# Another order of the stages of an attention pair, and the w_out loads issued by ScalarE

## The chip, the cores and the metric

The kernel runs on 1 core of one Trainium2 chip. The time is the device time of one execution in microseconds (us): 1208.38 us is the median of 3 runs of the kernel before (1195.93 to 1210.83). Everything that is said of its inside comes from one profiled execution of it.

## The reference

Three layers follow one another, all in float32.

- Attention over q, k, v of (4 batches, 8 heads, 768 tokens, 64): for each chunk of 32 queries, scores against 8 memory keys and a window of 56 keys, softmax, product with the values. Its output is laid out as 3072 tokens of 512.
- A gated layer: `sigmoid(x @ w_gate) * (x @ w_val) @ w_out`, with 512 to 1536 and back to 512.
- A rational layer: `h = x @ w_in` (512 to 2048), `g = P(h) / (Q(h) + 1e-6)` with P cubic and Q from |h| and h*h, then `g @ w_out`.

The output is (3072, 512) float32.

## The kernel before, in words

The engines run programs written out by hand, which meet at semaphores. Products that need full precision are made as three passes: each operand is split into a rounded part ("hi", a copy made by ScalarE) and the rest ("lo", a subtraction made by VectorE), and TensorE adds hi\*hi, hi\*lo and lo\*hi.

**Phases.** The tokens are worked off in NS = 3 stages of two blocks of 512 tokens. At the start, `attention(0)` runs alone on TensorE, with small products on the identity matrix between its parts (`warm_up`, L1117). Then comes for each stage s a run of six quads (`quad_a`, on TensorE two `chain` calls each), which make the gated layer's first products by a scheme with seven products (`STEPS`), and between the quads the thirds of the w_out products. Between two stages stands a **middle**: `attention(8 * (s + 1))` for the next tokens, with 30 of 36 remaining thirds of this stage between its parts, and the rest behind it. There are two middles. After the third stage the w_out products of the last blocks run while the weights of the rational layer are loaded and split (`split_b`), and then the rational layer runs to the end (`block_b`).

**An attention pair.** `attention` on TensorE (L1204) works off 8 units (a batch and half the heads' layout for 128 tokens each) in four pairs p = 0 to 3, with units a and b. For a unit there are: `scores` (64 small matmuls, L1086), on VectorE `softmax` without the exponent (a reduce L732, a subtract L735), on ScalarE `exp_scores` (L402), then the first `turn` (4 transposes, L1099), `copy_turned` on ScalarE (L408), `weigh_values` (64 small matmuls, L1111), on VectorE `normalize` (L743 to L747), the second `turn` (`turn(g, False)`), and `stage_x` on ScalarE (L418). `fill` is either one warm-up of three products or one third: four matmuls with 512 columns. Both units have buffers of their own; `scores` of unit g waits for `stage_x` of unit g - 2 (L1075).

**w_out pieces.** w_out is streamed as 72 pieces of 256 KB (12 per block), into a ring of ORING = 3 raw slots (`oraw`) and a ring of 3 split slots (`wout`). `load_oraw(n)` (L257) is issued by SyncE and waits until VectorE has made the lo part of piece n - 3 (`wo_lo`), since that reads the raw slot. `split_wout(n)` on ScalarE (L442) makes the hi part, on VectorE (L788) the lo part. A piece has three thirds on TensorE, and the first waits for its lo part (L1180). In the middles the pieces are split at the places that `at_middle(p, place)` names; on ScalarE place 0 lies between `copy_turned(a)` and `exp_scores(b)`, place 1 between that and `copy_turned(b)`, place 2 at the end of the pair. On VectorE place 0 lies between `softmax(a)` and `softmax(b)`, place 1 behind `normalize(a)`. `last_operands` splits what the next quads need, with three places `between(0)` to `between(2)` in which pieces n + 11 to n + 13 are split; n is the piece with which the middle begins.

SyncE's queue carries all transfers in program order: q, k and v of the units, the gated layer's weights (`load_raw`), the w_out pieces, the stores of finished blocks and the rational layer's weights.

Of the kernel before, what the change touches and what calls it, by code (L numbers as in the profile page):

```python
# [26 lines left out]
TA, TB = FA // P, FB // P  # L27
# [28 lines left out]
ORING = 3  # L56
# [12 lines left out]
def build(nc, q, k, v, wgv, wo, wb, coef_a, coef_b, y_dram, out):  # L69
    with ExitStack() as ctx:  # L70
# [168 lines left out]
        def _(sp):  # L239
# [58 lines left out]
            load_oraw(0)  # L298
            load_oraw(1)

            for s in range(NS):
                for i in range(NQ):
                    c, n = CHAINS * s + 2 * i, first_piece(s, i)
                    load_raw(c + 2)
                    load_oraw(n + 4)
# [7 lines left out]
                    load_oraw(n + 5)  # L313
# [6 lines left out]
                load_oraw(n + 4)  # L320
                load_qk(g + 2)
                load_oraw(n + 5)
                load_qk(g + 3)
                load_v(g + 2)
                store_a(2 * s, 0)
                store_a(2 * s, 1)
                load_oraw(n + 6)
                store_a(2 * s, 2)
                store_a(2 * s, 3)
                load_v(g + 3)  # L330
                for p in (1, 2):
                    load_qk(g + 2 * p + 2)
                    load_oraw(n + 2 * p + 5)
                    load_oraw(n + 2 * p + 6)
                    load_qk(g + 2 * p + 3)
                    load_v(g + 2 * p + 2)
                    load_v(g + 2 * p + 3)
                for ahead in range(11, 16):
                    load_oraw(n + ahead)
# [3 lines left out]
            load_oraw(n + 4)  # L343
            load_braw(B_EARLY + 1)
            load_oraw(n + 5)
# [4 lines left out]
            load_oraw(n + 6)  # L350
            for m in range(4):
                store_a(NT - 2, m)
            for ahead in range(7, TA + 2):
                load_braw(B_EARLY + ahead - 4)
                load_oraw(n + ahead)
# [42 lines left out]
        def _(act):  # L398
# [181 lines left out]

            attention(0, at_start)
            nc.scalar.preload_act_table_set("sigmoid_and_others")
# [7 lines left out]
            for s in range(NS - 1):  # L590
# [4 lines left out]
                def at_middle(p, place):  # L595
                    if place == 0:
                        split_wout(n + 2 * p + 2)
                        if p:
                            split_wout(n + 2 * p + 3)
                    if p == 0:  # L600
                        if place == 1:
                            copy_out_a(2 * s, 0)
                            copy_out_a(2 * s, 1)
                        elif place == 2:
                            split_wout(n + 3)
                            split_w(c, 0)
                    elif p == 1:
                        if place == 1:
                            split_w(c, 1)
                        elif place == 2:  # L610
                            split_w(c, 2)
                            split_w(c, 3)
                    elif p == 2:
                        if place == 2:
                            split_x(s + 1, B11)
                    elif place == 0:
                        split_x(s + 1, B21)
                    elif place == 2:
                        split_wout(n + 10)
                        split_x(s + 1, T2, 0)  # L620
# [4 lines left out]
                nc.scalar.preload_act_table_set("sigmoid_and_others")  # L625
# [101 lines left out]
        def _(dve):  # L727
# [168 lines left out]
            def last_operands(s, between):  # L896
                split_x(s, T2, 0)
# [3 lines left out]
                between(0)  # L901
# [470 lines left out]
```

## Time and profile before

| what | value |
|---|---|
| median of 3 runs | 1208.38 us (1195.93 to 1210.83) |
| the profiled execution, its own time | 1207.63 us |
| its span | 1205.3 us |
| TensorE busy | 1172.7 us (97%) |
| VectorE busy | 905.0 us (75%) |
| ScalarE busy | 751.3 us (62%) |
| GpSimd busy | 121.4 us (10%) |
| moved by DMA | 97.79 MB |

The span runs from the first to the last instruction; the time of the execution is 2.3 us longer. TensorE's busy time counts matmuls that overlap, so its idle time is read from single rows and not from the share. Its clock is shown as a share of full speed: 1.00 is 2.4 GHz and 0.50 is 1.2 GHz.

### The profile page before, as it was taken

Reading aid. Unit: us, or ns where it says so; the run is one execution under the profiler, and the core shown is the slowest. Engines: PE = TensorE matmul, PEld = TensorE weight load, DVE = VectorE, ACT = ScalarE, POOL = GpSimd, SP = SyncE. Lnnn points to the kernel's source line nnn. Section 1 sums busy time; section 2 is a strip of 40 time slices with the busy share of each in tenths; the row PEclk is TensorE's granted clock in tenths of the full one; section 3 lists DMA queues with packets and bytes.
Section 4 is the critical chain, followed back from the end, with each engine's and each line's share of the span. In section 5 each row is a group of like instructions: output and inputs, shape, how many; then the busy total and the mean of one; then the engine's idle time right before and its main releaser. Section 6 shows DMA issues by size and latency. Waiting matters only on the chain.

```text
span 1205.3 us, 21070 instructions
## 1 busy us (share of the span) xinstructions
PE 1172.7 (97%) x8160; PEld 962.8 (80%) x8160; DVE 905.0 (75%) x1387; ACT 751.3 (62%) x1224; POOL 121.4 (10%) x150
## 2 busy tenths in 40 slices
PE   8899999989999987999999999999999999999998
PEld 7778887768888765788887888888888888888887
DVE  3675666667566644676657899998998998988987
ACT  2464555455555533555555787777877877877875
POOL 2122222003322200223200000000000000000000
PEclk9999999999999998999999999999999999999999
DMA  8412422833242172332207400200200100100000
GB/s 285 150 53 79 141 70 71 277 100 110 79 140 79 63 246 100 99 133 84 90 24 248 171 1 1 70 1 1 70 0 0 70 0 0 70 0 0 36 1 35
DMA packets 40720, 97.79 MB, mean 81 GB/s; under 512 B 4288, under 2 KB 4288, under 8 KB 40640
## 3 DMA queue, kind: packets, MB, share of 16 engines
q1 hardware_dynamic: 40640, 96.68, 23.6%
q8 instruction: 55, 0.90, 0.3%
q14 instruction: 25, 0.20, 0.1%
HBM read 84.09 MB, written 12.58 MB: 80 GB/s over the span
## 4 chain that ended last, share of the span: by engine, by line
PE 91%; DVE 3%; ACT 2%; issue 2%; DMA 1%; SPq 0%; ACTq 0%; DVEq 0%
PE ps_h L1151 9%; PE ps_h L1158 9%; PE ps_h L1153 9%; PE ps_h L1257 7%; PE ps_h L1262 7%; PE ps_h L1258 7%; PE ps_y L1301 7%; PE ps_y L1295 7%; PE ps_y L1297 7%; PE ps_y L1196 4%; PE ps_y L1201 4%; PE ps_y L1197 4%; PE ps_h L1099 2%; PE ps_h L1086 1%; PE ps_h L1111 1%
## 5 line engine op out<-in xcount | busy, mean ns | idle before, releaser
L1151 PE MATMUL ps_h<-xop,wop 128*128 128x512 f32 x504 | 197.0, 391 | 1.8 <-DVE x_raw L806 1.5
L1153 PE MATMUL ps_h<-xop,wop 128*128 128x512 f32 x504 | 196.1, 389 | 0.0
L1158 PE MATMUL ps_h<-xop,wop 128*128 128x512 f32 x504 | 155.9, 390 | 0.0
L1257 PE MATMUL ps_h<-x_split,weights 128*128 128x512 f32 x384 | 149.4, 389 | 0.0
L1258 PE MATMUL ps_h<-x_split,weights 128*128 128x512 f32 x384 | 149.4, 389 | 0.0
L1295 PE MATMUL ps_y<-weights,hid 128*128 128x512 f32 x360 | 140.0, 389 | 0.0
L1297 PE MATMUL ps_y<-weights,hid 128*128 128x512 f32 x360 | 140.0, 389 | 0.0
L785 DVE TENSOR_TENSOR wop<-rawp,wop 128x448 fp32r<-128x448 f32 x144 | 91.3, 665 | 47.7 <-ACT wop L439 47.7
L1196 PE MATMUL ps_y<-hid,wout 128*128 128x512 f32 x264 | 109.9, 416 | 7.6 <-DVE wout L790 7.4
L806 DVE TENSOR_TENSOR x_raw<-ps_h,probs_t 128x512 f32<-128x512 f32 x72 | 49.5, 688 | 87.3 <-PE ps_h L1158 87.1
L672 ACT ACTIVATE tmp<-ps_h 128x512 f32<-128x512 f32 x96 | 57.1, 595 | 92.5 <-PE ps_h L1262 92.5
L1151 PEld LDWEIGHTS ps_h<-xop,wop 128*128 128x128 f32 x504 | 94.6, 188 | 23.4 <-DVE x_raw L806 2.4
L1153 PEld LDWEIGHTS ps_h<-xop,wop 128*128 128x128 f32 x504 | 94.7, 188 | 20.1
L1158 PEld LDWEIGHTS ps_h<-xop,wop 128*128 128x128 f32 x504 | 94.6, 188 | 19.7
L1197 PE MATMUL ps_y<-hid,wout 128*128 128x512 f32 x264 | 105.8, 401 | 0.0
L1262 PE MATMUL ps_h<-x_split,weights 128*128 128x512 f32 x384 | 102.6, 389 | 0.0
L1301 PE MATMUL ps_y<-weights,hid 128*128 128x512 f32 x360 | 96.2, 389 | 0.0
L1006 DVE TENSOR_TENSOR tmp<-tmp 128x512 f32<-128x512 f32 x96 | 66.1, 688 | 30.4 <-ACT tmp L675 30.4
L481 ACT ACTIVATE hid<-x_raw 128x512 fp32r<-128x512 f32 x72 | 45.4, 630 | 64.8 <-DVE x_raw L820 64.8
L790 DVE TENSOR_TENSOR wout<-oraw,wout 128x512 fp32r<-128x512 f32 x72 | 52.0, 730 | 44.2 <-ACT wout L446 44.2
L1257 PEld LDWEIGHTS ps_h<-x_split,weights 128*128 128x128 f32 x384 | 72.1, 188 | 15.0
L1262 PEld LDWEIGHTS ps_h<-x_split,weights 128*128 128x128 f32 x384 | 72.1, 188 | 15.0
(90 smaller groups left out, 2285.8 us busy)
## 6 DMA issues: line engine op xcount, KB each, us to landing
rawp<-wgv_l SPq DMA_DIRECT2D x36, 512.0 KB, 3.5
oraw<-wo_l SPq DMA_DIRECT2D x72, 256.0 KB, 3.6
unit<-v_l SPq DMA_DIRECT2D x24, 520.0 KB, 6.0
unit<-k_l SPq DMA_DIRECT2D x24, 512.0 KB, 5.6
unit<-q_l SPq DMA_DIRECT2D x24, 256.0 KB, 4.1
x_stage<-y_dram SPq DMA_DIRECT2D x6, 1024.0 KB, 5.8
out<-stage SPq DMA_DIRECT2D x24, 256.0 KB, 2.2
braw<-wb_l SPq DMA_DIRECT2D x11, 512.0 KB, 6.2
```

What stands on the lines that cost most here:

```text
L785: nc.vector.tensor_tensor(wop[:, c % 2, 1, cols], rawp[:, c % 2, 256 + 448 * i:256 + 448 * (i + 1)], wop[:, c % 2, 0, cols].bitcast(F32), ...
L1151: nc.tensor.matmul(dst, w_h[k], xop[:, m, 0, k, :], start=first and k == 0, stop=False, skip_group_check=True)
L1153: nc.tensor.matmul(dst, w_l[k], xop[:, m, 0, k, :], start=False, stop=False, skip_group_check=True)
L1158: last = nc.tensor.matmul(dst, w_h[k], xop[:, m, 1, k, :], start=False, stop=k == 1, skip_group_check=True)
L1196: nc.tensor.matmul(ps_y[:, m, :], w_at(0, m), h[0], start=f == 0, stop=False)
L1197: nc.tensor.matmul(ps_y[:, m, :], w_at(1, m), h[0], start=False, stop=False)
L1257: nc.tensor.matmul(dst, lhs(c, 0), x_split[:, 0, c, :], start=(c == 0), stop=False)
L1258: nc.tensor.matmul(dst, lhs(c, 1), x_split[:, 0, c, :], start=False, stop=False)
L1262: last = nc.tensor.matmul(dst, lhs(c, 0), x_split[:, 1, c, :], start=False, stop=(c == KT - 1))
L1295: nc.tensor.matmul(ps_y[:, m, :], hid_b(i, 0)[:, P * m:P * (m + 1)], wb_at(i, 1, 0), start=(i == 0), stop=False)
L1297: nc.tensor.matmul(ps_y[:, m, :], hid_b(i, 0)[:, P * m:P * (m + 1)], wb_at(i, 1, 1), start=False, stop=False)
L1301: nc.tensor.matmul(ps_y[:, m, :], hid_b(i, 1)[:, P * m:P * (m + 1)], wb_at(i, 1, 0), start=False, stop=False)
```

## The change

The order of a pair on TensorE: `scores(b)` follows directly on `turn(a, True)`; two fills stand between `scores(b)` and `weigh_values(a)`; `turn(a, False)` stands behind `weigh_values(b)`. The number of fills per pair stays. `load_oraw` moves from SyncE to ScalarE: pieces 0 and 1 are loaded first of all, and each `split_wout(n)` on ScalarE begins with `load_oraw(n + 2)`, wait included. The places of the splits in the middles change on ScalarE and VectorE, `between(0)` comes first in `last_operands`, and the load of the sigmoid table comes behind it.

```diff
@@ sync @@
-            def load_oraw(n):
-                if n >= PIECES:
-                    return
-                wait(sp, wo_lo, n - ORING + 1)
-                sp.dma_start(oraw[:, n % ORING, :], wo[n % TA]).then_inc(oraw_loaded[n % ORING], 16)
...  (all calls of load_oraw on SyncE are gone, the other issues keep their order)
@@ scalar @@
+            def load_oraw(n):
+                if n >= PIECES:
+                    return
+                wait(act, wo_lo, n - ORING + 1)
+                act.dma_start(oraw[:, n % ORING, :], wo[n % TA]).then_inc(oraw_loaded[n % ORING], 16)
+
             def split_wout(n):
+                load_oraw(n + 2)
                 act.wait_ge(oraw_loaded[n % ORING], 16 * (n // ORING + 1))
...
             def last_operands(s, between):
+                between(0)
+                nc.scalar.preload_act_table_set("sigmoid_and_others")
                 split_x(s, T3, 0)
                 split_x(s, T4, 0)
-                between(0)
...
+            load_oraw(0)
+            load_oraw(1)
             attention(0, at_start)
-            nc.scalar.preload_act_table_set("sigmoid_and_others")
...
                 def at_middle(p, place):
-                    if place == 0:
+                    if p < 2 and place == 0:
                         split_wout(n + 2 * p + 2)
-                        if p:
-                            split_wout(n + 2 * p + 3)
...
+                        split_wout(n + 2 * p + 3)
+                    elif p == 0 and place == 1:
+                        copy_out_a(2 * s, 0)
+                        copy_out_a(2 * s, 1)
+                    elif p == 0:
+                        split_w(c, 0)
+                    elif p == 1 and place == 1:
+                        split_w(c, 1)
                     elif p == 1:
+                        split_w(c, 2)
+                        split_w(c, 3)
+                        split_wout(n + 6)
+                    elif p == 2 and place == 0:
+                        split_wout(n + 7)
+                    elif p == 2 and place == 1:
+                        split_x(s + 1, B11)
                     elif p == 2:
+                        split_wout(n + 8)
+                        split_wout(n + 9)
                     elif place == 0:
                         split_x(s + 1, B21)
+                    elif place == 1:
                         split_wout(n + 10)
@@ vector @@
             def last_operands(s, between):
+                between(0)
                 split_x(s, T2, 0)
                 split_x(s, T1, 0)
                 token_sum(s, T3, 0)
                 token_sum(s, T4, 0)
-                between(0)
...
                 def at_middle(p, place):
                     if place == 0:
                         split_wout(n + 2 * p + 2)
-                        if p:
-                            split_wout(n + 2 * p + 3)
+                        split_wout(n + 2 * p + 3)
+                        if p == 3:
+                            token_sum(s + 1, T1, 0)
...
@@ tensor @@
                     turn(a, True)
-                    fill()
                     scores(b)
-                    weigh_values(a)
                     fill()
                     fill()
+                    weigh_values(a)
                     turn(b, True)
-                    turn(a, False)
+                    fill()
                     fill()
                     weigh_values(b)
+                    turn(a, False)
                     fill()
```

## Rows read from the trace of the kernel before

**Rows 1.** Windows: us, busy us (instructions) of each engine, TensorE clock, DMA share, GB/s.
```profile
0.00:60.00 60.00, 50.51 (x1301) 46.06 (x1302) 30.56 (x56) 23.39 (x39) 10.88 (x18) 0.97 0.66 218
211.00:291.00 80.00, 76.24 (x1255) 60.27 (x1254) 52.63 (x91) 41.11 (x74) 7.40 (x8) 0.98 0.49 167
421.00:515.00 94.00, 81.11 (x1254) 63.28 (x1253) 52.86 (x93) 41.31 (x73) 6.99 (x8) 0.93 0.44 147
642.00:680.00 38.00, 37.60 (x164) 30.16 (x163) 30.55 (x35) 26.68 (x37) 0.00 (x0) 1.00 0.78 279
```
**Rows 2.** Waits, whole span: who waited for whom, us in total, times, longest.
```profile
PE ps_y L1196 <- DVE wout L790: 7.4, 5, 1.9
PE ps_h L1111 <- issue: 7.4, 4, 3.5
PE ps_h L1086 <- issue: 7.0, 3, 3.6
```
**Rows 3.** TensorE's timeline, first middle: start, us, and the idle time before.
```profile
234.37 0.60 PE L1099 MATMUL ps_h<-ident,probs 128*128 128x128 f32 x4
237.27 0.50 PE L1196 MATMUL ps_y<-hid,wout 128*128 128x512 f32 x1
239.50 1.09 PE L1099 MATMUL ps_h<-ident,probs 128*128 128x128 f32 x8
243.38 1.14 PE L1086 MATMUL ps_h<-unit 64*32 64x64 f32 x64
249.39 0.50 PE L1196 MATMUL ps_y<-hid,wout 128*128 128x512 f32 x1 [1.93 <-DVE wout L790]
264.85 0.50 PE L1196 MATMUL ps_y<-hid,wout 128*128 128x512 f32 x1 [1.64 <-DVE wout L790]
```
**Rows 4.** ScalarE's timeline in the same pair.
```profile
235.01 0.60 ACT L408 ACTIVATE probs_t<-ps_h 128x512 f32<-128x512 f32 x1 [0.36 <-PE ps_h L1099]
235.50 1.14 ACT L446 ACTIVATE wout<-oraw 128x512 fp32r<-128x512 f32 x2
238.81 0.63 ACT L402 ACTIVATE probs<-probs 128x512 f32<-128x512 f32 x1 [2.17 <-DVE probs L735]
```
**Rows 5.** VectorE's timeline in the same pair, and a lo pair before it.
```profile
223.99 1.29 DVE L790 TENSOR_TENSOR wout<-oraw,wout 128x512 fp32r<-128x512 f32 x2 [2.66 <-ACT wout L446]
236.16 1.29 DVE L790 TENSOR_TENSOR wout<-oraw,wout 128x512 fp32r<-128x512 f32 x2 [2.66 <-ACT wout L446]
237.37 0.68 DVE L732 TENSOR_REDUCE row_stats<-ps_h 128x8 f32<-128x512 f32 x1
238.09 0.69 DVE L735 TENSOR_TENSOR probs<-ps_h,row_stats 128x512 f32<-128x512 f32 x1
```
**Rows 6.** SyncE's queue, first middle: issues and how long each held the queue.
```profile
212.84 0.33 SPq L261 DMA_DIRECT2D oraw<-wo_l  x1
213.69 1.77 SPq L244 DMA_DIRECT2D unit<-k_l  x1
224.71 0.93 SPq L261 DMA_DIRECT2D oraw<-wo_l  x2
```
**Rows 7.** TensorE's timeline, start and second middle: stalls named issue, the first wait.
```profile
5.78 0.85 PE L1086 MATMUL ps_h<-unit 64*32 64x64 f32 x64 [1.32 <-DMA unit<-k_l]
38.61 0.30 PE L1111 MATMUL ps_h<-unit,probs_t 64*32 64x65 f32 x2 [3.53 <-issue]
433.95 0.63 PE L1086 MATMUL ps_h<-unit 64*32 64x64 f32 x37 [3.60 <-issue]
475.63 0.43 PE L1111 MATMUL ps_h<-unit,probs_t 64*32 64x65 f32 x25 [2.31 <-issue]
```
**Rows 8.** Windows of 2 us, columns as in the first group.
```profile
251.00:253.00 2.00, 2.00 (x97) 1.73 (x94) 1.62 (x4) 0.00 (x0) 0.00 (x0) 0.50 0.61 224
265.00:267.00 2.00, 2.00 (x9) 1.65 (x10) 1.21 (x3) 0.78 (x2) 0.00 (x0) 1.00 0.53 126
432.00:434.00 2.00, 0.05 (x7) 0.05 (x11) 0.00 (x0) 0.00 (x0) 0.00 (x0) 1.00 1.03 391
436.00:438.00 2.00, 2.00 (x9) 1.71 (x8) 0.04 (x1) 1.23 (x2) 0.00 (x0) 0.50 0.95 344
```
**Rows 9.** TensorE's timeline, start: the two first turns of the second pair.
```profile
21.50 0.66 PE L1099 MATMUL ps_h<-ident,probs 128*128 128x128 f32 x4 [0.20 <-ACT probs L402]
25.96 1.09 PE L1099 MATMUL ps_h<-ident,probs 128*128 128x128 f32 x8 [0.15 <-ACT probs L402]
```

More of the change, by code:

```diff
@@ L319, in _ @@
                 n, g = piece_of(s, 0, TA - 2), UNITS * (s + 1)
-                load_oraw(n + 4)
                 load_qk(g + 2)
-                load_oraw(n + 5)
                 load_qk(g + 3)
                 load_v(g + 2)
[L325 to L329, printed above, removed]
-                load_v(g + 3)
[L331 to L339, printed above, removed]
+                for m in range(4):
+                    store_a(2 * s, m)
+                load_v(g + 3)
+                load_qk(g + 4)
+                load_qk(g + 5)
+                load_v(g + 4)
+                load_v(g + 5)
+                load_qk(g + 6)
+                load_qk(g + 7)
+                load_v(g + 6)
+                load_v(g + 7)
             n = piece_of(NS - 1, 0, TA - 2)
             load_braw(B_EARLY)
-            load_oraw(n + 4)
             load_braw(B_EARLY + 1)
-            load_oraw(n + 5)
             for m in range(4):
@@ L349, in _ @@
             load_braw(B_EARLY + 2)
-            load_oraw(n + 6)
             for m in range(4):
                 store_a(NT - 2, m)
-            for ahead in range(7, TA + 2):
-                load_braw(B_EARLY + ahead - 4)
-                load_oraw(n + ahead)
+            for o in range(B_EARLY + 3, TB - 1):
+                load_braw(o)
             load_braw(TB - 1)
@@ L595, in at_middle @@
                 def at_middle(p, place):
-                    if place == 0:
+                    if p < 2 and place == 0:
                         split_wout(n + 2 * p + 2)
-                        if p:
-                            split_wout(n + 2 * p + 3)
[L600 to L606, printed above, removed]
-                    elif p == 1:
[L608 to L612, printed above, removed]
+                        split_wout(n + 2 * p + 3)
[6 more added lines that the diff above has]
+                        split_w(c, 1)
+                    elif p == 1:
+                        split_w(c, 2)
[5 more added lines that the diff above has]
+                        split_x(s + 1, B11)
                     elif p == 2:
-                        if place == 2:
-                            split_x(s + 1, B11)
+                        split_wout(n + 8)
+                        split_wout(n + 9)
                     elif place == 0:
                         split_x(s + 1, B21)
-                    elif place == 2:
+                    elif place == 1:
                         split_wout(n + 10)
+                    else:
                         split_x(s + 1, T2, 0)
@@ L958, in at_middle @@
                     else:
+                        token_sum(s + 1, T2, 0)
                         split_x(s + 1, B21)
                         split_wout(n + 10)
-                    if p == 3 and place == 0:
-                        token_sum(s + 1, T1, 0)
-                        token_sum(s + 1, T2, 0)
                 attention(UNITS * (s + 1), at_middle)
```

8 lines of the change are left out of this document (1 added, 7 removed).

## The prediction

> **What bounds the kernel now.** I read the windows by stage first, then the table of waits, then TensorE's timeline of the start and the middles beside those of ScalarE, VectorE and SyncE's queue. TensorE is the bound nearly everywhere: from 642 to 680 us it idles 0.4 us [rows 1], and in the rational layer behind 680 us, which the change does not touch, it runs back to back. What the change can reach is the start (60 us, 9.5 us idle), the first middle (80 us, 3.8 idle) and the second (94 us, 12.9 idle, at a mean clock of 0.93) [rows 1]. The two middles hold the same instructions, so the 14 us between them are stalls. Three kinds of idle time make up most of it [rows 2]: 7.4 us in which a third waits for the lo part of its w_out piece, and 14.4 us of "issue", in which TensorE stands still inside its runs of 64 small matmuls with nothing to wait for: 7.4 us in `weigh_values` (4 times) and 7.0 us in `scores` (3 times). An idle stretch costs twice: after the 1.93 us one [rows 3] the clock stands at 0.50, that is 1.2 GHz, and after the 3.60 us one [rows 7] too [rows 8]. Each such stretch at 1.2 GHz lasted about 4 us, so about 2 us are lost each time. After the 1.64 us idle time [rows 3] the clock stayed at 1.00 [rows 8]. I take the price of an idle stretch over 1.9 us as itself plus up to 2 us.
>
> The sum is made against the profiled execution, 1207.63 us, which is 0.75 us below the median.
>
> **The pair on TensorE.** Stage lengths from the first middle, start to start: a turn 0.36 us, scores or weigh before a fill 0.78, a fill about 1.03, or 1.1 before small matmuls. Between the first turn of a and the first turn of b TensorE now has a fill, scores, weigh and two fills, and the pair takes 5.13 us there (234.37 to 239.50 [rows 3]), the last half microsecond of it waiting. Changed, it has 0.36 + 0.78 + 1.03 + 1.10 + 0.78 = 4.05 us of work there: one fill less. The chain that runs beside it on the other engines is what decides. From the same rows: turn a to `copy_turned` 0.64, copy to the first hi 0.49 [rows 4], that to the first lo 0.66, two lo parts to the reduce 1.21, reduce to subtract 0.72, subtract to exp 0.72, exp to the turn of b 0.69 [rows 3 to 5]. That is the 5.13 us.
>
> **The new wait.** In p = 0 and p = 1 ScalarE splits two pieces at place 0, and the second `split_wout(m + 1)` now begins with `load_oraw(m + 3)`, which waits for the lo part of piece m. So hi, lo, hi, lo run one behind the other instead of overlapping. Queued behind that wait on ScalarE are the second hi and exp(b); VectorE waits for the hi with softmax(b) behind it, and TensorE's turn of b waits for exp(b). SyncE's issue came 0.72 us after the start of the lo part (223.99 to 224.71 [rows 5, 6]) and held its queue 0.33 us [rows 6]; the trace has no issue on ScalarE, so I take that. The chain becomes 0.64 + 0.49 + 0.66 + (0.72 + 0.37) + 0.66 + 0.60 + 0.72 + 0.72 + 0.69 = 6.27 us, and TensorE idles 2.2 us. From the turn of b to the next pair it then has 0.36 + 1.0 + 1.1 + 0.78 + 0.36 + 1.1 = 4.7 us. So p = 1 takes 10.97 us from the turn of a, against 8.99 now (about +2.0), and p = 0, where one piece is split now, +2.2. In p = 2 one hi is left in the chain: 4.52 us against 4.05, +0.2 for the pair.
>
> **What the other places give back.** In p = 3 the pieces' hi parts are made in p = 2 already, so the 1.93 us wait and its half clock go: the stretch from turn a to the last turn was 13.0 us and becomes 9.65, -3.35. With `between(0)` first, piece n + 11 is ready and the 1.64 us wait goes: -1.8 with what lay around it. Per middle 2.2 + 2.0 + 0.2 - 3.35 - 1.8 = -0.75, for both -1.5. The four new idle stretches of 2.2 us may each be followed by half clock: 0 to 8 us, since 1.64 us left the clock alone and 1.93 did not. I take half, +3.8.
>
> **The start.** Warm-ups cover the waits there. The first turn of a to that of b is 4.46 us (21.50 to 25.96 [rows 9]) and has one split in it; TensorE's new work is about 3.55, so 0.9 us of waiting, 0.15 of it there already, in two pairs, and 0.5 in the last: +2.0. The two w_out loads that ScalarE issues at once add 0.5 MB to the first burst, before the q and k loads for which TensorE already waits 1.32 us [rows 7]. At the 391 GB/s of a full stretch [rows 8] that is 1.3 us at most, 0 at least; I take +1.2, since both loads are in flight when the first scores need k.
>
> **Moves at no price.** In the quads ScalarE gets 0.33 us per issue, six microseconds apart, beside the idle time in which it waits for TensorE; without that cover it would be up to 50 x 0.33 = 16 us. The loads are issued two pieces ahead, about 8 us in the middles against a landing of some 3.6 us; behind 642 us TensorE needs 5.4 us for two pieces, and 0.3 us of wait may go or come. SyncE loses 72 issues, and none of its q, k, v loads waits behind a `wo_lo` wait any longer; v of a comes one and a half microseconds later by the later weigh, but is needed a pair later. The table load moves behind one more split and keeps two steps of the first chain as cover. Scores of the next a now stand only a fill behind `turn(a, False)`: 0.36 + 1.1 us against 0.64 + 0.6 + 0.1 for `stage_x`, no wait, by 0.1 us.
>
> **The issue stalls.** The long ones end as a burst of transfers drains (391 GB/s from 432 to 434 us [rows 8]), and the instructions between two neighbouring ones come to about 256, so I read them as the fetch of the next block of instructions. Four of the seven lie in `weigh_values` directly behind `scores`, where 256 instructions go by in 1.44 us. Changed, no two of these runs touch, and 256 instructions take 2.9 us at least. I count these four as gone: 0.96 + 3.53 + 0.55 + 2.31 = 7.35 us and 4 us of half clock behind two of them, -11.3. Bounds: nothing gone, 0; all seven gone, 7.0 us and some 5.5 us of half clock more, -24.
>
> The Trainium skill ("Runtime: NRT & Kernel Launch", Instruction fetch mechanics) says that TensorE's instruction memory is refilled in 16 KiB blocks of 256 instructions, that it holds 2048, and that crossing a block is mostly hidden. By that the spacing of two runs would not matter, and the -11.3 would be 0; the trace agrees on the 256 and not on the hiding, with stalls of 3.5 us.
>
> **Sum.** 1207.63 - 1.5 + 3.8 + 2.0 + 1.2 - 11.3 = 1201.8, so 1202 us.
>
> **Rivals.** (1) The stalls go by the bursts alone, and stay: the first middle had a busy DMA and none, which speaks for chance; that `weigh_values` behind `scores` has four of seven speaks weakly against. 1202 + 11.3 = 1213 us. (2) All seven go, since the new idle stretches give the fetch time: 1202 - 12.5 = 1189 us. (3) The new wait on ScalarE does not bite, because the second issue runs ahead of what I assume: 1202 - 4 x 2.2 - 3.8 = 1189 us; with rival 2 on top 1177, over 2% faster. The wait is in the program and its lo part in the trace, which speaks against. (4) Slower than before: ScalarE's issues are held up as SyncE's was for 1.77 us [rows 6], in the four serial chains at place 0, and each is followed by half clock while the stalls stay. 1213 + 4 x 1.44 + 3.8 = 1223 us; it decides against the forecast once an issue takes over 1.3 us (or over 0.33 with the stalls kept). For over 2% slower both middles must also stall as the second does now (+14): 1237. The Trainium skill ("DMA: Bandwidth & Descriptors", Arbitration) says that each DMA engine takes turns between the queues that have work for it; that would bring the w_out loads past the k and v bursts, and by it this rival would lose its ground, but an own landing time of a ScalarE load is in no row here.
>
> **Chances.** Forecast 0.40 (1195 to 1208 by itself), rival 1 0.27, rival 2 0.13, rival 3 0.10, rival 4 0.10. The range 1187 to 1217 holds the first four but for the meeting of 2 and 3, and leaves out rival 4. A difference of 2%, 24 us, is about what a measurement of this kernel can tell from no change: faster by over 2% 0.05, slower 0.04, within 0.91.
>
> **What would show it.** Right: the turn of b follows the turn of a by about 6.3 us in p = 0 and 1 of both middles, with some 2.2 us of idle time put down to exp; no wait for wout in p = 3 and behind the attention; ScalarE's own queue with issues of 0.33 us; no issue stall in `weigh_values`. Wrong: issue stalls as long as before at other places; no idle time at the turn of b; a first `scores` at the same 5.78 us; waits in the quads for `snapshot` copies, which would mean that ScalarE's issues are not covered.

## The result and the profile after

The changed kernel is slower: 1209.22 us median of 20 runs (1205.3 to 1213.09), against 1201.44 us of 20 runs of the kernel before (1195.93 to 1210.95). The ratio is 1.0054, interval 1.0036 to 1.0073. The forecast was 1202 us and a range up to 1217: the time lies in the range, the direction was wrong.

The two profiled executions show the opposite, 1207.63 us before and 1205.3 after. That is the first thing to see: the profiled execution of before stood 6 us above the median that more runs gave, and the sum was made against it. That of the changed kernel stood 4 us below its median and is the fastest of its 20 runs, so what the two profiles show side by side flatters the change by 10 us. The page of the changed kernel:

```profile
span 1202.9 us, 21070 instructions
PE 1169.1 (97%) x8160; PEld 957.6 (80%) x8160; DVE 901.8 (75%) x1387; ACT 752.5 (63%) x1224; POOL 118.7 (10%) x150
q10 hardware_dynamic: 10368, 18.88, 5.1%
oraw<-wo_l ACTq DMA_DIRECT2D x72, 256.0 KB, 2.7
```

The w_out loads have a queue of their own (q10) and land after 2.7 us instead of 3.6. The windows of the start and the two middles, columns as in [rows 1]:

```profile
0.00:60.00 60.00, 48.74 (x1278) 42.96 (x1279) 27.16 (x52) 21.65 (x36) 9.18 (x18) 1.00 0.65 214
211.00:291.00 80.00, 72.79 (x1242) 56.21 (x1241) 49.24 (x86) 38.92 (x68) 6.45 (x8) 1.00 0.53 172
421.00:515.00 94.00, 83.78 (x1342) 64.63 (x1341) 58.96 (x102) 44.15 (x77) 8.08 (x8) 0.98 0.49 159
```

The waits over the whole span, which answer to [rows 2]:

```profile
PE ps_h L1087 <- ACT probs L382: 15.8, 17, 2.1
PE ps_y L1184 <- DVE wout L780: 2.3, 1, 2.3
PE ps_h L1087 <- DVE probs L737: 2.3, 3, 1.5
```

The issue stalls sum to 3.6 us where they were 14.4, the waits for wout to 2.3 where they were 7.4; in their place stand 15.8 us of waiting for exp (1.8 before). From TensorE's timelines, first scores to first chain: the first middle went from 61.8 to 63.4 us, the second from 76.0 to 66.0 (it had the long stalls), the start to the first chain from 60.3 to 62.9, the six quads between the middles from 148.3 to 149.3, and all behind the second middle from 713.2 to 715.8. The six quads ahead of the first middle took 145.6 us in both. So each stretch that the change reaches got longer except the one in which that execution of before had stalled most.

### The profile page after: what moved, and what is told of

Same layout as the page of the kernel before. It is cut to its first block, busy times and chain, and to the rows that moved or that the text cites. A ratio compares the mean times of both kernels' runs of the same rounds, so it can differ in the third digit from the quotient of the medians.

```text
span 1202.9 us, 21070 instructions
## 1 busy us (share of the span) xinstructions
PE 1169.1 (97%) x8160; PEld 957.6 (80%) x8160; DVE 901.8 (75%) x1387; ACT 752.5 (63%) x1224; POOL 118.7 (10%) x150
## 4 chain that ended last, share of the span: by engine, by line
PE 90%; DVE 5%; ACT 3%; issue 2%; DMA 0%; ACTq 0%; SPq 0%; DVEq 0%
PE ps_h L1139 9%; PE ps_h L1146 9%; PE ps_h L1141 9%; PE ps_h L1245 7%; PE ps_h L1250 7%; PE ps_h L1246 7%; PE ps_y L1283 7%; PE ps_y L1289 7%; PE ps_y L1285 7%; PE ps_y L1184 4%; PE ps_y L1185 4%; PE ps_y L1189 4%; PE ps_h L1087 2%; PE ps_h L1099 1%; PE ps_y L1107 1%
## 5 line engine op out<-in xcount | busy, mean ns | idle before, releaser
L775 DVE TENSOR_TENSOR wop<-rawp,wop 128x448 fp32r<-128x448 f32 x144 | 88.4, 644 | 58.2 <-ACT wop L419 58.2
L1184 PE MATMUL ps_y<-hid,wout 128*128 128x512 f32 x264 | 107.3, 406 | 2.5 <-DVE wout L780 2.3
L1185 PE MATMUL ps_y<-hid,wout 128*128 128x512 f32 x264 | 104.3, 395 | 0.0
L1246 PEld LDWEIGHTS ps_h<-x_split,weights 128*128 128x128 f32 x384 | 72.1, 188 | 15.0
L1250 PEld LDWEIGHTS ps_h<-x_split,weights 128*128 128x128 f32 x384 | 72.1, 188 | 15.0
L1245 PEld LDWEIGHTS ps_h<-x_split,weights 128*128 128x128 f32 x384 | 72.0, 188 | 14.9
```

What stands on the lines that cost most here:

```text
L775: nc.vector.tensor_tensor(wop[:, c % 2, 1, cols], rawp[:, c % 2, 256 + 448 * i:256 + 448 * (i + 1)], wop[:, c % 2, 0, cols].bitcast(F32), ...
L1184: nc.tensor.matmul(ps_y[:, m, :], w_at(0, m), h[0], start=f == 0, stop=False)
L1185: nc.tensor.matmul(ps_y[:, m, :], w_at(1, m), h[0], start=False, stop=False)
L1245: nc.tensor.matmul(dst, lhs(c, 0), x_split[:, 0, c, :], start=(c == 0), stop=False)
L1246: nc.tensor.matmul(dst, lhs(c, 1), x_split[:, 0, c, :], start=False, stop=False)
L1250: last = nc.tensor.matmul(dst, lhs(c, 0), x_split[:, 1, c, :], start=False, stop=(c == KT - 1))
```

## The new waits, each in its rows

**Hi, lo, hi, lo in series.** TensorE in the first middle: the first turn of a and that of b in pair 1, the first turn of a in pair 3, the last turn, and the first chain.

```profile
227.19 0.60 PE L1087 MATMUL ps_h<-ident,probs 128*128 128x128 f32 x4
233.53 0.66 PE L1087 MATMUL ps_h<-ident,probs 128*128 128x128 f32 x4 [2.12 <-ACT probs L382]
256.13 0.65 PE L1087 MATMUL ps_h<-ident,probs 128*128 128x128 f32 x4 [1.24 <-ACT probs L382]
265.90 0.60 PE L1087 MATMUL ps_h<-ident,probs 128*128 128x128 f32 x4
271.84 0.39 PE L1139 MATMUL ps_h<-xop,wop 128*128 128x512 f32 x1
```

The turns stand 6.34 us apart (6.40 in pair 0) against 5.13 in [rows 3], with 2.12 us of idle time. ScalarE and its queue (ACTq) in the same pair:

```profile
227.82 0.60 ACT L388 ACTIVATE probs_t<-ps_h 128x512 f32<-128x512 f32 x1 [0.35 <-PE ps_h L1087]
227.83 0.33 ACTq L426 DMA_DIRECT2D oraw<-wo_l  x1
228.32 0.62 ACT L433 ACTIVATE wout<-oraw 128x512 fp32r<-128x512 f32 x1
229.70 0.33 ACTq L426 DMA_DIRECT2D oraw<-wo_l  x1
230.13 0.63 ACT L433 ACTIVATE wout<-oraw 128x512 fp32r<-128x512 f32 x1 [1.19 <-DVE wout L780]
232.85 0.63 ACT L382 ACTIVATE probs<-probs 128x512 f32<-128x512 f32 x1 [2.08 <-DVE probs L725]
```

VectorE in the same pair, the first lo part:

```profile
228.97 0.69 DVE L780 TENSOR_TENSOR wout<-oraw,wout 128x512 fp32r<-128x512 f32 x1 [2.65 <-ACT wout L433]
```

The first issue runs beside the copy and costs nothing. The second comes at 229.70 us, only when VectorE has made the lo part (228.97 to 229.66), and the second hi stands behind it; in [rows 4] both hi parts ran back to back.

**Exp of pair 3.** ScalarE at the end of pair 2 (first middle), where `split_wout(n + 9)` was put:

```profile
254.50 0.33 ACTq L426 DMA_DIRECT2D oraw<-wo_l  x1
254.93 0.63 ACT L433 ACTIVATE wout<-oraw 128x512 fp32r<-128x512 f32 x1 [3.09 <-PE ps_y L1189]
255.47 0.61 ACT L382 ACTIVATE probs<-probs 128x512 f32<-128x512 f32 x1
```

The issue of piece n + 11 waits for the lo part of n + 8, which VectorE makes behind softmax(a) of pair 3 (253.78 to 254.46 us), and exp(a) stands behind it: the 1.24 us wait at 256.13 above. The row names TensorE as releaser, but the issue that holds the hi part back came less than 0.1 us behind VectorE's lo part.

**The start.** First rows of ScalarE, then of VectorE, between the second and the third pair, then of TensorE: the first scores, the two turns at the third pair, and the last turn of all:

```profile
32.15 0.60 ACT L398 ACTIVATE x_raw<-ps_h 128x512 f32<-128x512 f32 x1 [2.12 <-PE ps_h L1087]
32.65 0.57 ACT L419 ACTIVATE wop<-rawp 128x448 fp32r<-128x448 f32 x1
```
```profile
33.25 0.63 DVE L775 TENSOR_TENSOR wop<-rawp,wop 128x448 fp32r<-128x448 f32 x1 [4.02 <-ACT wop L419]
34.83 0.68 DVE L722 TENSOR_REDUCE row_stats<-ps_h 128x8 f32<-128x512 f32 x1
```
```profile
6.60 1.17 PE L1074 MATMUL ps_h<-unit 64*32 64x64 f32 x64 [2.13 <-DMA unit<-k_l]
34.97 0.66 PE L1087 MATMUL ps_h<-ident,probs 128*128 128x128 f32 x4 [0.41 <-DVE probs L737]
36.95 0.66 PE L1087 MATMUL ps_h<-ident,probs 128*128 128x128 f32 x4 [0.66 <-ACT probs L382]
59.83 0.66 PE L1087 MATMUL ps_h<-ident,probs 128*128 128x128 f32 x4 [1.51 <-DVE probs L737]
```

`turn(a, False)` now stands behind `weigh_values(b)`, so `stage_x(a)` on ScalarE comes late, and behind it in program order the hi part of the gated layer's weights. VectorE has the matching lo part in front of `normalize(b)` and of the next `softmax`. So the later turn costs at the next pair's two turns (0.41 and 0.66 us), on engines where nothing had moved. In the kernel before the same chain had ended in time: ScalarE's `stage_x(a)`, VectorE's lo part, and TensorE's turn of the last b with no wait, then that of a:

```profile
27.14 0.59 ACT L418 ACTIVATE x_raw<-ps_h 128x512 f32<-128x512 f32 x1
28.23 0.62 DVE L785 TENSOR_TENSOR wop<-rawp,wop 128x448 fp32r<-128x448 f32 x1 [1.95 <-ACT wop L439]
30.86 0.60 PE L1099 MATMUL ps_h<-ident,probs 128*128 128x128 f32 x4
32.34 0.66 PE L1099 MATMUL ps_h<-ident,probs 128*128 128x128 f32 x4 [0.20 <-ACT probs L402]
```

The last turn waits 1.51 us for `normalize` (0.60 before). The first scores come at 6.60 us instead of 5.78 [rows 7].

**Behind the second middle.** TensorE in the first chain of the last quads:

```profile
492.32 0.50 PE L1184 MATMUL ps_y<-hid,wout 128*128 128x512 f32 x1 [2.29 <-DVE wout L780]
493.90 0.50 PE L1139 MATMUL ps_h<-xop,wop 128*128 128x512 f32 x1 [0.37 <-ACT probs_t L440]
```

The wait for piece n + 11 behind the attention (1.64 us in [rows 3]) is gone, and TensorE reaches piece n + 12 earlier, which waits for the same row of splits and sums on VectorE and ScalarE. Behind the second middle the gain is given back, and 1 us more. Behind the first no wait for wout came; a wait of 0.39 us stands in its first quad, and the six quads take 1.0 us more, so part of the gain stays there.

## The experiments

Each ratio is against runs of the kernel before on the same chip. Differences between experiments go by ratios; 0.001 is 1.2 us. The changed kernel has 20 runs, e7 and e9 have 8, e11 and e12 have 6, the others 12. The last column is the distance from the lowest run to the median; it depends on the number of runs, and for the kernel before it was 5.5, 6.3, 7.5 and 4.7 us in the other comparisons. The standard deviation is steadier: 4.2 to 5.0 us for the kernel before in each comparison, 2.0 for the changed one.

| kernel | median us | ratio and interval | lowest to median |
|---|---|---|---|
| before (35 runs of one comparison) | 1203.48 | | 9.8 |
| changed | 1209.22 | 1.0054 (1.0036 to 1.0073) | 3.9 |
| e1 order only | 1207.77 | 1.0028 (1.0006 to 1.0051) | 2.1 |
| e2 loads only | 1202.98 | 0.9985 (0.9960 to 1.0009) | 4.8 |
| e3 first loads late | 1207.46 | 1.0042 (1.0016 to 1.0067) | 2.6 |
| e4 load behind hi | 1200.98 | 0.9981 (0.9950 to 1.0012) | 3.0 |
| c1 before again | 1203.78 | 1.0000 (0.9969 to 1.0031) | 5.8 |
| e5 old order at the start | 1203.14 | 0.9987 (0.9960 to 1.0014) | 3.5 |
| e6 loads on SyncE | 1197.62 | 0.9983 (0.9961 to 1.0004) | 1.1 |
| e7 before, earlier splits | 1196.79 | 0.9924 (0.9893 to 0.9955) | 7.1 |
| e8 e7, loads on ScalarE | 1195.32 | 0.9947 (0.9923 to 0.9971) | 3.9 |
| e9 small loads | 1192.60 | 0.9941 (0.9918 to 0.9964) | 0.7 |
| e10 runs apart, same cover | 1201.27 | 0.9979 (0.9953 to 1.0005) | 6.6 |
| e11 e7 and e10 | 1190.49 | 0.9913 (0.9885 to 0.9942) | 2.0 |
| e12 changed, e3 + e4 + e5 | 1195.90 | 0.9891 (0.9848 to 0.9933) | 4.7 |
| e13 changed, piece n + 9 later | 1208.37 | 1.0015 (0.9987 to 1.0043) | 3.5 |

**e1, the order alone.** Only TensorE's pair order of the changed kernel, in the kernel before.

> The kernel before with TensorE's new pair order alone (loads on SyncE, splits where they were). Theory A (the new order has one fill too few between the two first turns, 4.05 us of work for a chain of 5.13 us, and the issue stalls are small in a typical run): about 1.1 us of wait for exp at the turn of b in p = 1 to 3 of both middles, +0.6 us a pair net, some +3.5 us in the start; +6 us against before in all. Rival B (the order pays, because the issue stalls shrink, and the cost of the change lies in ScalarE's loads): no slower than before, -3 to 0 us, and fewer issue stalls in the profile.

Slower by 3.4 us of the forecast 6. The sign speaks against rival B: the order does not pay by itself. Its profile has 9.4 us of waiting for exp in all and 8.8 us of issue stalls, fewer than the 14.4 of before, as rival B had said.

**e2, the loads alone.** `load_oraw` on ScalarE in front of each split, in the kernel before.

> The kernel before with the w_out loads issued by ScalarE alone (old pair order, splits where they were). Theory A (the load in front of the second of two neighbouring splits waits for the first one's lo part, so hi, lo, hi, lo run in series): the turn of b comes 6.3 us after the turn of a in p = 1 to 3 instead of 5.13, +1.2 us each, +7 us, and +2 us at the start from the two first loads; +9 us. Theory C (the issues themselves on ScalarE cost, 0.33 us x 72, wherever they stand): waits of TensorE spread over the quads as well, and more than +9. Rival B: +9 too. Rival D (the order alone is what costs): 0 to +2 us.

Measured -1.8 us, no difference, where theory A said +9. The mechanism is there: the turns stand 6.34 us apart in pairs 1 and 2, and the first middle takes 64.65 us instead of 61.81. But the old order had 5.1 us of cover, so only 1.33 us of each 6.34 is idle. In its profile the waits for exp rose by 5.6 us (7.4 against 1.8; some 7 were forecast), and the issue stalls were 8.9 us against 14.4. So the serial wait is there, and something of nearly its size came back. That the own queue is what brings the stalls down is not shown: e8 has the same queue and 12.4 us of them.

**e3, the first two loads late.**

```diff
-            load_oraw(0)
-            load_oraw(1)
             attention(0, at_start)
+            load_oraw(0)
+            load_oraw(1)
```

> The changed kernel, with the loads of pieces 0 and 1 issued behind the first attention instead of ahead of it. Theory A (0.5 MB of w_out share the DMA engines with the first q and k): first scores back at 5.8 us instead of 6.6, no half clock behind it, -2 us against the changed kernel. Rival: the first scores are as late without them, by the landing of k alone, 0 us.

The first scores came at 5.25 us instead of 6.60. They came at 6.16 to 6.60 us in the five profiles in which ScalarE loads pieces 0 and 1 first of all, and at 5.01 to 5.78 in the eleven others, so the mechanism is shown; the time went from 1.0054 to 1.0042, 1.4 us, inside the intervals.

**e4, the load behind the hi part.**

```diff
             def split_wout(n):
-                load_oraw(n + 2)
                 act.wait_ge(oraw_loaded[n % ORING], 16 * (n // ORING + 1))
...
                 nc.scalar.activation(wout[:, n % ORING, 0, :], oraw[:, n % ORING, :], ACT.Copy).then_inc(wo_hi, 1)
+                load_oraw(n + 2)
```

> The changed kernel, with load_oraw(n + 2) behind the hi part of split_wout(n) instead of in front of it: the same issues and the same semaphore, but no hi part stands behind the wait. Theory A (serial chain): the turn of b follows the turn of a by 5.1 to 5.3 us in p = 0 and 1 instead of 6.34 to 6.40, so 4 x 1.1 = -4.5 us against the changed kernel; the 1.24 us wait in p = 3 stays, since exp(a) still stands behind the load of n + 11. Theory C (issue time as such): 0 us, the waits stay at 2.1 us.

From 1.0054 to 0.9981: one moved line gives 8.8 us. TensorE's two turns of pair 1 in the first middle:

```profile
230.31 0.60 PE L1087 MATMUL ps_h<-ident,probs 128*128 128x128 f32 x4
235.43 0.66 PE L1087 MATMUL ps_h<-ident,probs 128*128 128x128 f32 x4 [0.93 <-ACT probs L382]
```

5.12 us, as forecast, with the same 72 issues on ScalarE: issuing there costs nothing, the wait in front of the hi part does. The four chains give 4.9 us, and the wait in pair 3, which was expected to stay at 1.24, fell to 0.71 and 0.65 us, 1.1 us more. Some 3 us are left over. A part of it is the clock. In the changed kernel the first such wait of the second middle (2.11 us, ending at 431.94 us) is followed by half clock, the one of the first middle is not:

```profile
430.00:432.00 2.00, 0.06 (x1) 0.06 (x2) 1.90 (x5) 0.74 (x2) 0.00 (x0) 1.00 1.01 359
434.00:436.00 2.00, 2.00 (x47) 1.25 (x51) 0.50 (x1) 0.00 (x0) 0.00 (x0) 0.50 0.97 371
```

So an idle stretch of 2.1 us sometimes costs itself alone and sometimes 1.7 us more. The changed kernel, e3, e5 and e13 have four such waits each in pairs 0 and 1 of their middles: 7 of these 16 were followed by half clock, 1, 2, 2 and 2. In e4's middles no wait for exp is above 0.93 us and none is followed by half clock; its 2.27 us wait for piece n + 12, behind the second middle, is.

**c1, the kernel before again.**

> The kernel before against itself: a ratio of 1.00 within its interval, and a second profile of it. Theory S (its issue stalls are a lottery of each run: its runs spread from 1193.7 to 1216.3 us, and the profiled one stood high in them): the second profile has issue stalls at other places or of another sum than 14.4 us, and the first middle and the other stages agree with the first profile to 0.3 us where no stall falls. Rival: the stalls sit at fixed places in every run, and the same seven come back.

The ratio is 1.0000. Its issue stalls, from TensorE's timeline:

```profile
37.24 0.30 PE L1111 MATMUL ps_h<-unit,probs_t 64*32 64x65 f32 x2 [2.72 <-issue]
245.38 0.34 PE L1086 MATMUL ps_h<-unit 64*32 64x64 f32 x13 [2.28 <-issue]
256.58 0.54 PE L1111 MATMUL ps_h<-unit,probs_t 64*32 64x65 f32 x35 [1.19 <-issue]
427.66 0.34 PE L1111 MATMUL ps_h<-unit,probs_t 64*32 64x65 f32 x12 [0.56 <-issue]
436.92 0.87 PE L1086 MATMUL ps_h<-unit 64*32 64x64 f32 x37 [2.79 <-issue]
466.49 0.30 PE L1086 MATMUL ps_h<-unit 64*32 64x64 f32 x4 [3.17 <-issue]
477.71 0.66 PE L1111 MATMUL ps_h<-unit,probs_t 64*32 64x65 f32 x25 [1.62 <-issue]
```

Half right and half wrong for both sides. Where a stall comes is fixed: a run stops with 2, 37 and 25 of its 64 matmuls to go, just as in [rows 7]. Whether it comes, and how long it lasts, is not: the first middle has two here and had none, two of the start are missing. The sum is 14.3 us again, and this profiled execution (1210.18 us) too stood 6 us above the median of its kernel.

Two more readings tell what these stalls are. Counted in matmuls from the first, the stalls of the start come behind number 222, 349, 858 or 985, in all 16 profiles and in every order of the pair. They are 127 or 509 matmuls apart; 127 matmuls with their weight loads are 254 instructions, and a few waits stand between them. And each page of the profile lists a queue for instructions (packets, MB, share of the DMA engines), here that of before, and the same queue from 431.5 to 432.0 us, inside the 3.60 us stall of [rows 7]:

```profile
q8 instruction: 55, 0.90, 0.3%
q8 instruction: 1, 0.02, 11.9%
```

These are 55 packets of 16 KB. The one in that stall ran from 431.61 to 432.57 us, and TensorE went on at 433.95. All 94 stalls named issue in the 16 profiles end 1.1 to 1.7 us after such a packet has landed. So the stalls are waits for the next block of instructions, which the prediction had only read from the counts. The packets behind these stalls took 0.9 to 1.5 us, one took 2.3. A long stall is one whose packet started late: that of the 3.60 us stall started 1.26 us after TensorE had stopped. Why it starts late is open.

**e5, the old order at the start.** `attention` takes the old order for `first == 0`.

> The changed kernel with the old pair order in the first attention alone. Theory A (the new order has one warm-up too few over each chain, and the waits for exp and for normalize add up to 6.2 us in the profile of the changed kernel against 1.4 before): the start shortens by 4 to 5 us, and so does the time. Rival (the start is set by the landing of q, k and v, whatever the order): 0 to -1 us.

From 1.0054 to 0.9987, 8 us (6 by medians), more than theory A's 4 to 5, and the first chain starts at 56.76 us instead of 62.92. Of these 6.2 us, 0.2 lie ahead of the first scores and 0.5 in issue stalls. The forecast had +2.0 us for the order there.

**e6, the loads back on SyncE**, with order and places as changed.

> The changed kernel with the w_out loads back on SyncE at the places where the kernel before issues them; TensorE's order and the places of the splits as changed. Theory A: both serial waits on ScalarE go, turn a to turn b 5.1 to 5.3 us in p = 0 and 1, no 1.24 us wait in p = 3, and the first scores come at 5.0 to 5.8 us; -7 us and more against the changed kernel, 1201 to 1203 us. Rival (the order's missing fill is nearly the whole cost): at most -3 us, 1206 and above.

0.9983 and 1197.62 us: -8.5 us. More than what the changed kernel loses against before (6.5 us) goes with the load in ScalarE's queue in front of the hi part, and e4 gets the same back without moving the loads away. The rival is out. But e5 gets as much back at the start, so this is not the only cause: the changed kernel carries both costs, and its gains elsewhere cover one of them.

**e7, the kernel before with earlier splits.** Only what the change does well: piece n + 8 at the end of pair 2, `between(0)` first.

```diff
                     if place == 0:
-                        split_wout(n + 2 * p + 2)
+                        if p < 3:
+                            split_wout(n + 2 * p + 2)
...
                     elif p == 2:
-                        if place == 2:
+                        if place == 1:
                             split_x(s + 1, B11)
+                        elif place == 2:
+                            split_wout(n + 8)
```

> The kernel before (order and loads untouched) with the two late pieces split earlier: piece n + 8 at the end of pair 2, between(0) first in last_operands with the table load behind it. Theory A: the 1.93 us wait and the 2 us of half clock behind it go in both middles, and that is kept, -7 us; the 1.64 us wait goes from its place, but comes back in the first chain of the next quads as a wait for piece n + 12, 0 us. Rival (what was forecast): the 1.64 us are kept as well, -11 us.

-9.1 us by the ratio, -7.0 by medians, between the two theories and settling neither. The first middle takes 58.8 us instead of 61.8, and the quads behind it 0.4 us more; all behind the second middle takes 2.4 us more (715.6 against 713.2). That speaks for theory A, though not by a wait at piece n + 12: the waits for wout are 0.9 us in all.

**e8, e7 with the loads behind the hi part on ScalarE.**

> The kernel before with the earlier splits of e7, and the w_out loads issued by ScalarE behind each hi part, the first two behind the first attention. Theory A (the issue itself is covered, and only hi parts queued behind the load's wait cost; the own queue thins out the bursts, so fewer issue stalls): 1193 to 1196 us, narrower spread than e7. Theory C (issues on ScalarE cost as such): above 1199 us.

1195.3 us as theory A said, but by the ratio no better than e7 (0.9947 and 0.9924, intervals overlapping), and with 12.4 us of issue stalls in its profile against 10.5 in that of e7. That the own queue gives fewer stalls is not borne out.

**e9, small loads.** From the third unit on only 64 columns of q, k and v are loaded.

> The kernel before, which from the third unit on loads only 64 columns of q, k and v (so it computes with old data; the program and all semaphores are the same). Theory F2 (issue stalls are instruction fetches held up by bursts of data on the same DMA engines): no stall above 0.3 us in the profile, the half clock behind them gone, the runs within 2 to 3 us of each other at 1193 us or a little below, -9 us against before. Rival (the fetch itself is too slow for 256 instructions in 1.44 us, whatever else moves): the stalls come back at their places, and the spread stays.

It runs at 1192.6 us within 4 us from lowest to highest. Its stalls in the second middle, and, with columns as in [rows 1], the microsecond in which TensorE stops for the last:

```profile
419.20 0.34 PE L1113 MATMUL ps_h<-unit,probs_t 64*32 64x65 f32 x12 [0.69 <-issue]
426.54 0.63 PE L1088 MATMUL ps_h<-unit 64*32 64x64 f32 x37 [0.87 <-issue]
451.95 0.30 PE L1088 MATMUL ps_h<-unit 64*32 64x64 f32 x4 [0.46 <-issue]
462.12 0.44 PE L1113 MATMUL ps_h<-unit,probs_t 64*32 64x65 f32 x25 [2.57 <-issue]
459.00:460.00 1.00, 0.55 (x50) 0.38 (x38) 0.82 (x2) 0.00 (x0) 0.00 (x0) 1.00 0.88 330
```

The same four places. Two are far shorter (3.60 to 0.87 us, 2.62 to 0.46), two are not (0.55 and 0.69, 2.31 and 2.57). In front of the longest one the DMA engines are busy all the same (share 0.88, 330 GB/s): two w_out loads, which were not made smaller, run there, and the block of instructions starts at 459.63 us. So the bursts of q, k and v lengthen the stalls and make them vary; they do not make them. Without them the kernel is 7 us faster, of which the profile shows 8.5 us less of stalls than in before (5.9 against 14.4). Both theories were too simple.

**e10, the runs apart with the same cover.**

```diff
                     turn(a, True)
                     fill()
                     scores(b)
-                    weigh_values(a)
-                    fill()
                     fill()
+                    weigh_values(a)
+                    fill()
                     turn(b, True)
-                    turn(a, False)
                     fill()
+                    turn(a, False)
                     weigh_values(b)
```

> The kernel before with one edit on TensorE: in a pair the three fills between the two first turns are dealt out as fill, scores(b), fill, weigh(a), fill, so that the two runs of 64 small matmuls do not touch but the work between the turns stays 4.6 us and more. Theory F (issue stalls are instruction fetches that cannot keep up with 256 instructions in 1.44 us beside a burst of transfers): the spread of its runs narrows to that of the changed order (2 to 5 us from the lowest to the median instead of 10) with the lowest at 1194 to 1196, so a median of some 1198, -5 us. Rival G (the stalls go by the bursts alone): same median and spread as before. Rival H (they shrank in the changed kernel only because TensorE idled more and gave the fetch its time): same as before too, but the order alone, with its waits, had less.

-2.5 us with an interval that holds zero: inconclusive. The stalls in its profile are 10.0 us, 1.7 of them in `weigh_values` (7.4 in before) and 8.3 in `scores` (7.0), and the places in the start are again behind matmuls 349, 858 and 985. That the neighbourhood of the two runs makes the stalls, on which -11.3 us of the forecast rested, is not shown: where they come goes by the count.

**e11, e7 and e10 together.**

> The kernel before with the earlier splits of e7 and the fills dealt out as in e10. If the two gains add: 1196.8 - 2.5 = 1194 us. If what e10 gave was chance: 1197 us. If normalize or the lo parts are pushed into each other by both: above 1198 us, with a wait for wout in p = 3.

1190.49 us, 0.9913 (0.9885 to 0.9942): faster than both kernels, 1.4% below the changed one. Against e7 the intervals overlap, so whether e10's part adds is open. Its profile, taken in the slowest of its six runs, has 7.1 us of issue stalls, that of e7 10.5.

**e12, three mends together**: e3, e4 and e5 in the changed kernel.

> The changed kernel with three of its parts undone or mended together: the load behind the hi part (as in e4), the old pair order in the first attention (as in e5), the first two loads behind that attention (as in e3). Theory A (three separate waits that add up: -8.2, -6.1 and -1.8 us by medians against the changed kernel): some 1193 to 1196 us, below the kernel before. Rival (they overlap, one hides the other, for instance since any idle time lets the instruction fetch catch up and its loss brings issue stalls back): 1199 to 1202 us, and more issue stalls in its profile than the changed kernel's 3.6 us.

0.9891 (0.9848 to 0.9933). Against the changed kernel this is -0.0163; the three single steps give -0.0012, -0.0073 and -0.0067, together -0.0152. Within the intervals they add. The changed kernel without these three is faster than the one before. Its profile has 7.1 us of issue stalls against 3.6 in the changed one, as the rival had it; one profile each does not tell whether that is more than chance.

**e13, piece n + 9 later.**

> The changed kernel with one split moved in the middles on ScalarE: piece n + 9 from the end of pair 2 to place 0 of pair 3, so that exp(a) of pair 3 no longer stands behind the load of piece n + 11, which waits for the lo part of n + 8. Theory A: the 1.24 us wait at the first turn of a in p = 3 goes in both middles, and nothing takes its place, -2.5 us against the changed kernel. Rival (the chain is only moved: hi of n + 9 and the B21 split now stand before exp(b)): the wait comes back at the turn of b in p = 3, 0 us.

The wait at the first turn of a goes, and this stands at that of b in pair 3, first middle (1.67 us in the second):

```profile
266.19 0.66 PE L1087 MATMUL ps_h<-ident,probs 128*128 128x128 f32 x4 [1.45 <-ACT probs L382]
```

By the rows the rival is right, the wait is moved. The ratio (1.0015) lies lower than the changed kernel's, with intervals that just overlap; I go by the rows.

## Why the prediction was wrong, point by point

The steps that failed: the credit for stalls was counted on an execution 6 us above the typical one, the order in the start was priced at a third of its cost, and three waits were put at nothing, those in front of the first turn of a in pairs 2 and 3 and that at piece n + 12.

- **The profiled execution as the base: wrong.** The sum started at 1207.63 us. More runs put the median at 1201.44, and the three runs shown (1195.93 to 1210.83) had said that single executions differ by 15 us. Both profiles of this kernel, with 14.4 and 14.3 us of stalls, come from executions 6 us above their medians. A credit for stalls taken from one high execution is only worth what the typical one has of them.
- **The new wait in pairs 0 and 1: right in size.** 6.27 us forecast, 6.40 and 6.34 measured, 2.2 us of idle time forecast and 2.1 measured, the issue of 0.33 us right. Half clock behind half of these was right too: 7 of 16 in four profiles.
- **Pair 2 from the turn of a on: right** (9.31 us to the next scores, 9.01 before; +0.2 forecast).
- **What the other places give back: the step that failed in the middles.** Turn a to the last turn takes 9.77 us (9.65 forecast), and from turn a of pair 3 to the chain it is 5.16 us less than before in the first middle, 5.15 forecast. But the text priced each pair from turn a on and did not ask what stood in front of it. From scores(a) to the first turn of a pair 2 takes 3.98 us (3.18 before) with a wait of 0.41, and pair 3 takes 4.58 (3.48 before) with the 1.24 us behind the load of n + 11: 1.9 us in the first middle, and the same two waits stand in the second. So the first middle became 1.5 us longer, where the sum had -0.75 ahead of its +3.8 for half clock, and none of its new waits was followed by half clock in this profile. And the 1.64 us came back as 2.29 and 0.37 us at piece n + 12 behind the second middle; what is late next was not looked for.
- **The start: mis-sized by a factor of about three.** The order was put at +2.0 us, e5 shows 6 to 8 by the runs and 5.4 by the rows. The waits for exp at the turn of b were right (0.68, 0.66). Missed was that a later `turn(a, False)` delays `stage_x`, behind it a weight split, behind that on VectorE `normalize` and the next softmax. The move was followed on TensorE and not through the queues of the other two engines. The first loads were put at +1.2 us; the first scores came 0.8 us later, e3 gives 1.4.
- **The issue stalls: right in direction, its reason not shown.** The idle time went from 14.4 to 3.6 us in the two profiles, more than the 7.35 forecast, but these two flatter it. The six profiles with the new order throughout have 3.6, 8.8, 4.3, 6.0, 7.4 and 4.0 us (changed, e1, e3, e4, e6, e13), mean 5.7; the five with the old order and full loads 14.4, 14.3, 8.9, 10.5 and 12.4 (before, c1, e2, e7, e8), mean 12.1. So some 6 us went, near the forecast, and that they are waits for instructions is shown. Why fewer come is not: TensorE also idles more in the new order (rival 2), and e10, the clean test of the 256 instructions in 1.44 us, is inconclusive. The Trainium skill ("Runtime: NRT & Kernel Launch", Instruction fetch mechanics) says that block crossings are mostly hidden; the trace disagrees where runs of 64 small matmuls cross one, with stalls of up to 3.6 us.
- **ScalarE's issues as such cost nothing: right** (e4: the same issues, 8.8 us less). Rival 3, that the wait does not bite, is out; so is rival 4, its issues held 0.33 us. Rival 2 has its stalls nearly gone in this one profile, but not its time. The time lies nearest to rival 1, for other reasons than it gave.

In one sentence: the forecast was 6 us faster and the kernel came out 8 us slower; 6 us of this way are the base, and the waits that the sum missed (about 4 us in the start, the same in front of pairs 2 and 3 of both middles, 2.7 behind the second) are the rest. The parts are read from single executions and come to a little more than the whole, so their sizes are good to some microseconds only.

## What to carry to other kernels

A load that waits for a slot belongs behind the work that its engine does next, not in front: the same issue on the same queue cost 8.8 us in front, and behind it the time was that of e6, where the loads were moved away (0.9981 and 0.9983). When a stage is moved on the bound engine, follow its consumer through the program order of every other engine, to the first instruction on which the bound engine waits; that is where the price shows, often one pair later. And before a stall of one profiled execution is credited to a change, look at the spread of the runs: what varies from run to run is not all there to be had.

## What the runs showed of the hardware

- TensorE can wait for its own instructions: all 94 stalls named issue in the 16 profiles end 1.1 to 1.7 us after a 16 KB packet of the instruction queue has landed. Where such a stall can come is fixed by the count of instructions; whether it comes and how long it lasts (up to 3.60 us here) differs from one execution to the next, and two of the four in the second middle got far shorter with small q, k and v loads (rows of c1, e9 and [rows 7]).
- A DMA issue on ScalarE held its queue 0.33 us and ran beside the activation in front of it (227.82 and 227.83 us above); it held nothing up where its semaphore was already there.
- Loads of 256 KB on a queue of their own landed after 2.7 to 2.8 us in the median (eight profiles), against 3.5 to 3.6 in the shared one (eight profiles).
- An idle stretch of 2.1 us left TensorE's clock at 1.00 in the first middle of the changed kernel and was followed by 0.50 in the second; over four profiles 7 of 16 such stretches were followed by it.
